# One attention phase on one core: a second load queue, a short first inverse, zeroing on GpSimd, and a new order of SyncE's work

## What is computed

```python
for t in range(S):
    y[:, :, t] = np.einsum('bhd,bhde->bhe', rt, state)
    Sa = np.einsum('bhde,bhe->bhd', state, at)
    state_decay = state * wt[:, :, None, :] - np.einsum('bhd,bhe->bhde', Sa, bt)
    state = state_decay + np.einsum('bhd,bhe->bhde', vt, kt)
```

## Time and profile before

| | us |
|---|---|
| median of 3 runs | 957.0 (953.57 to 958.44) |
| the profiled execution, its own time | 948.12 |
| its span, first to last instruction | 946.4 |
| TensorE busy | 801.0 (85%) |
| VectorE, ScalarE, GpSimd busy | 516.9, 384.4, 270.3 |

### The profile page before, as it was taken

The page is one execution under the profiler, slowest core; times in us unless marked ns, Lnnn a source line. Parts: engine busy times, 40 slices in busy tenths (PEclk is TensorE's granted clock), DMA queues, the critical chain, the costliest instruction groups (busy, mean ns, idle before and its releaser), DMA issues.

```text
span 946.4 us, 29782 instructions
## 1 busy us (share of the span) xinstructions
PE 801.0 (85%) x13477; PEld 740.6 (78%) x13477; DVE 516.9 (55%) x703; ACT 384.4 (41%) x511; POOL 270.3 (29%) x412
## 2 busy tenths in 40 slices
PE   2887299898998987778509998999989998999987
PEld 2776288787888876667508998999988998999987
DVE  5898076675756631222356348554476446763484
ACT  1222044443434333434336127652466317571264
POOL 1039881955918728200002020030201220020200
PEclk9987599999989896998858999999989999999999
DMA  9776565857555245341440000100101001010001
GB/s 104 116 119 107 82 93 121 121 96 132 96 89 98 52 95 154 69 68 32 138 140 1 1 21 14 59 1 1 34 1 59 1 1 34 17 43 1 1 1 42
DMA packets 229097, 58.04 MB, mean 61 GB/s; under 512 B 219728, under 2 KB 224364, under 8 KB 228972
## 3 DMA queue, kind: packets, MB, share of 16 engines
q1 hardware_dynamic: 202860, 52.21, 27.9%
q10 hardware_dynamic: 26112, 3.94, 2.8%
HBM read 41.96 MB, written 14.16 MB: 59 GB/s over the span
## 4 chain that ended last, share of the span: by engine, by line
PE 39%; DVE 5%; ACT 3%; DMA 2%; issue 1%; SPq 0%; DVEq 0%; ACTq 0%
PE pp L802 37%; DVE stage L1070 3%; PE pp L882 2%; ACT stage L975 1%; DVE w L990 1%; DVE big L990 1%; ACT stage L970 1%; DMA tmp<-in_moe_w_in_dram 1%; DMA rows_raw<-in_moe_conv_w_dram 1%; DMA tmp<-x_scratch 1%; ACT w L920 0%; ACT tmp L967 0%; SPq L729 0%; DMA out_dram<-stage 0%; ACT stage L985 0%
## 5 line engine op out<-in xcount | busy, mean ns | idle before, releaser
L246 POOL TENSOR_TENSOR prod<-t_pair 128x30 f32<-128x30 f32 (+9 forms) x180 | 105.0, 583 | 149.7 <-DMA t_pair<-m_scratch 135.9
L802 PE MATMUL pp<-xs,w 128*128 128x384 f32 x640 | 117.2, 339 | 0.2
L802 PEld LDWEIGHTS pp<-xs,w 128*128 128x128 f32 x640 | 112.8, 189 | 1.8 <-ACT stage L967 1.5
L249 POOL TENSOR_TENSOR t_pair<-t_pair,prod 128x30 f32<-128x30 f32 (+9 forms) x180 | 109.2, 607 | 14.1
L802 PE MATMUL pp<-wo,big 128*128 128x320 f32 x576 | 96.0, 327 | 13.0 <-DVE big L990 12.4
L802 PEld LDWEIGHTS pp<-wo,big 128*128 128x128 f32 x576 | 91.9, 201 | 16.0 <-issue 13.6
L802 PE MATMUL pp<-wsg,big 128*128 128x384 f32 x576 | 102.0, 338 | 0.0
L802 PEld LDWEIGHTS pp<-wsg,big 128*128 128x128 f32 x576 | 101.4, 188 | 0.0
L1088 POOL TENSOR_TENSOR big<-stage,big 128x1024 fp32r<-128x1024 f32 x12 | 28.8, 2397 | 253.7 <-DVE stage L1034 253.7
L348 DVE TENSOR_TENSOR ar_sb<-p,mask 128x512 f32<-128x512 f32 x24 | 16.6, 691 | 107.1 <-PE p L492 107.1
L802 PE MATMUL pp<-w,xs 128*128 128x512 f32 x192 | 47.6, 409 | 27.2 <-DVE xs L990 27.2
(11 more groups left out here) (128 smaller groups left out, 1479.3 us busy)
## 6 DMA issues: line engine op xcount, KB each, us to landing
vp<-in_v_dram ACTq DMA_DIRECT2D x96, 40.0 KB, 3.0
raw_r<-in_r_dram SPq DMA_DIRECT2D x48, 80.0 KB
x_scratch<-y_t SPq DMA_DIRECT2D x48, 80.0 KB
out_dram<-stage SPq DMA_DIRECT2D x12, 320.0 KB, 2.3
m_scratch<-n_t SPq DMA_DIRECT2D x48, 64.0 KB
t_pair<-m_scratch SPq DMA_DIRECT2D x6, 512.0 KB, 4.0
t_scratch<-t_pair SPq DMA_DIRECT2D x6, 512.0 KB, 4.4
t_sb<-t_scratch SPq DMA_DIRECT2D x24, 128.0 KB, 3.5
```

Source lines behind the costliest of these rows:

```text
L246: pool.tensor_tensor(p_v, tp[:, 0:s, s:s + 1].to_broadcast([PAIRS, s, n]), tp[:, s:s + 1, s + 1:C].to_broadcast([PAIRS, s, n]), ALU.mult). ...
L249: pool.tensor_tensor(tp[:, 0:s, s + 1:C], tp[:, 0:s, s + 1:C], p_v, ALU.add).then_inc(elim, 1)
L802: last = pe.matmul(out_of(p, half), l, r, start=step == 0 and first, stop=step == steps - 1 and not part)
```

## The change

It has four parts. (1) SyncE and ScalarE both load in the lead-in: k and a of the first two pairs of units and k of pairs 2 to 4 go out on ScalarE's queue, SyncE no longer waits for `padded`, and v's first loads go out in steps 5 and 6. (2) The sets are cut otherwise: set 0 holds units 0 and 1 only, the following ones four units each (2 to 5, 6 to 9, ...), the last one two, seven sets in place of six. Set 0 has 64 matrices, and each is split over two partitions, even rows on one and odd rows on the other. (3) GpSimd zeroes z, vp and r_t, and ScalarE the edge of w_back. (4) SyncE's list is put in another order: its iteration s now serves unit s - 1, beginning with the wait for that unit's n_t. LAG stays at 9. The diff, cut to its core:

```diff
+        SETS = NU // 4 + 1
+        T_OUT = [0] + [32 + 16 * g for g in range(SETS)]
+        M_IN = [0] + [64 + 16 * g for g in range(SETS)]
+        HEAD = 5
+        def set_of(u):
+            return (u + 2) // 4, (u + 2) % 4
+        def last_unit(g):
+            return min(4 * g + 1, NU - 1)
+        def first_chunk(g):
+            return max(4 * g - 2, 0)
+        t_first = free(s_sb[:], 0, [[C, C // 2], [1, C]])
         @block.sync
-            sp.wait_ge(padded, 9)
             load(w, "w", 0, w_in)
-            load(k, "k", 0, k_in)
             load(b, "b", 0, b_in)
-            load(a, "a", 0, a_in)
             load(w, "w", 1, w_in)
-            load(k, "k", 1, k_in)
             load(b, "b", 1, b_in)
-            load(a, "a", 1, a_in)
             load_r(0)
-            for s in STEPS:
+            for s in range(NC + LAG + 2):
+                u = unit(s - 1)
+                if u is not None:
+                    g, at = set_of(u)
+                    sp.wait_ge(n_done, 2 * u + 2)
...
+                    for be in range(2):
+                        n0 = be * HP + at * 16 if g else be * C + u * 16
+                        sp.dma_start(m_pairs[n0:n0 + 16].rearrange("n s t -> s n t"),
+                                     n_t[be * HP + C:be * HP + 2 * C, u % RN].rearrange("p j x t -> p (j x) t")).then_inc(m_out, 16)
+                    if u == last_unit(g):
+                        sp.wait_ge(m_out, (u + 1) * 32)
...
+                        if g == 0:
+                            for half in range(2):
+                                rows = slice(half * HP, (half + 1) * HP)
+                                sp.dma_start(t_first[rows], m_pairs[0:HP].rearrange("n (i x) t -> x n i t", x=2)[half]).then_inc(m_in, 16)
+                                sp.dma_start(t_pair[rows, 0], m_pairs[0:HP]).then_inc(m_in, 16)
+                        else:
+                            sp.dma_start(t_pair[:, g % 2], m_pairs).then_inc(m_in, 16)
+                for g in range(SETS):
+                    if s != first_chunk(g) + LAG - (1 if g else 2):
+                        continue
+                    sp.wait_ge(elim, ELIM[g + 1])
...
+                        sp.dma_start(t_pairs, t_pair[:, g % 2]).then_inc(t_out, 16)
+                    sp.wait_ge(t_out, T_OUT[g + 1])
...
+                cy = chunk(s - LAG - 2)
+                if cy is not None and cy % 2 == 1:
+                    sp.wait_ge(y_done, cy + 1)
...
+                        sp.dma_start(rows, y_t[bi * HP:bi * HP + D, :, be, :]).then_inc(y_out, 16)
                 if u is not None:
                     if u % 2 == 0 and u // 2 + 2 < NU // 2:
                         sp.wait_ge(w_full, u + 2)
                         load(w, "w", u // 2 + 2, w_in)
                     if u % 2 == 1 and u // 2 + 2 < NU // 2:
-                        sp.wait_ge(k_full, u + 1)
-                        load(k, "k", u // 2 + 2, k_in)
+                        if u // 2 + 2 >= HEAD:
+                            sp.wait_ge(k_full, u + 1)
+                            load(k, "k", u // 2 + 2, k_in)
                         sp.wait_ge(b_full, u + 1)
                         load(b, "b", u // 2 + 2, b_in)
                         sp.wait_ge(a_full, u + 1)
                         load(a, "a", u // 2 + 2, a_in)
-                ur = unit(s - R_LAG)
+                ur = unit(s - 1 - R_LAG)
                 if ur is not None and ur + 1 < NU:
                     sp.wait_ge(r_full, ur + 1)
                     load_r(ur + 1)
...
         @block.gpsimd
+            pool.wait_ge(mask_step, 5)
+            pool.memset(z[:], 0.0).then_inc(blank, 1)
+            pool.memset(vp[:], 0.0).then_inc(blank, 1)
+            pool.memset(r_t[:], 0.0).then_inc(blank, 1)
+            pool.wait_ge(m_in, M_IN[1])
+            for s in range(1, C - 1):
+                n, m = C - 1 - s, (s + 1) // 2
...
+                pool.tensor_tensor(p_v, t_first[:, 0:m, s:s + 1].to_broadcast([P, m, n]),
+                                   t_pair[:, 0, s:s + 1, s + 1:C].to_broadcast([P, m, n]), ALU.mult).then_inc(elim, 1)
...
         @block.scalar
+            load_side(k, "k", 0, k_in)
+            load_side(a, "a", 0, a_in)
             act.wait_ge(mask_step, 5)
-            for c in range(RV):
-                load_v(c)
+            act.activation(w_back[:, :, C - 1:C], mask[:, 0:16].rearrange("p (n o) -> p n o", o=1), ACT.Copy, scale=0.0)
...
+                if s == -1:
+                    load_side(k, "k", 1, k_in)
+                if s == 0:
+                    load_side(a, "a", 1, a_in)
+                if 5 <= s < 5 + RV:
+                    act.wait_ge(blank, 3)
+                    load_v(s - 5)
+                if 0 < s and s % 2 == 1 and s // 2 + 2 < HEAD:
+                    act.wait_ge(k_full, s + 1)
+                    load_side(k, "k", s // 2 + 2, k_in)
         @block.vector
-            dve.memset(w_back[:, :, C - 1:C], 0.0).then_inc(const_done, 1)
-            dve.memset(vp[:], 0.0)
-            dve.memset(r_t[:], 0.0)
-            dve.memset(z[:], 0.0).then_inc(const_done, 1)
         @block.tensor
-            pe.wait_ge(const_done, 4)
+            pe.wait_ge(padded, 9)
```

More of the change, by code:

```diff
@@ L147, in _ @@
             load(w, "w", 0, w_in)
-            load(k, "k", 0, k_in)
             load(b, "b", 0, b_in)
-            load(a, "a", 0, a_in)
             load(w, "w", 1, w_in)
-            load(k, "k", 1, k_in)
             load(b, "b", 1, b_in)
-            load(a, "a", 1, a_in)
             load_r(0)
-            for s in STEPS:
[L157 to L162, removed]
+            for s in range(NC + LAG + 2):
[3 more added lines that the diff above has]
+                    sp.wait_ge(n_done, 2 * u + 2)
+                    if g and at == 0:
+                        sp.wait_ge(m_in, M_IN[g])
+                    for be in range(2):
[4 more added lines that the diff above has]
+                        sp.wait_ge(m_out, (u + 1) * 32)
+                        if g >= 2:
+                            sp.wait_ge(t_out, T_OUT[g - 1])
+                        if g == 0:
[5 more added lines that the diff above has]
+                            sp.dma_start(t_pair[:, g % 2], m_pairs).then_inc(m_in, 16)
+                for g in range(SETS):
+                    if s != first_chunk(g) + LAG - (1 if g else 2):
+                        continue
+                    sp.wait_ge(elim, ELIM[g + 1])
+                    if g == 0:
+                        for half in range(2):
+                            sp.dma_start(t_pairs[0:HP].rearrange("n (i x) t -> x n i t", x=2)[half],
+                                         t_first[half * HP:(half + 1) * HP]).then_inc(t_out, 16)
+                    else:
@@ L173, in _ @@
+                cy = chunk(s - LAG - 2)
+                if cy is not None and cy % 2 == 1:
+                    sp.wait_ge(y_done, cy + 1)
+                    for be, bi in SIDES:
+                        rows = x_t[2 * bi + be].rearrange("(h e) s -> e h s", e=D)[:, :, (cy - 1) * C:(cy + 1) * C]
+                        sp.dma_start(rows, y_t[bi * HP:bi * HP + D, :, be, :]).then_inc(y_out, 16)
                 if u is not None:
@@ L191, in _ @@
                     load_r(ur + 1)
[L192 to L213, removed]
+                if s == NU + 1:
+                    sp.wait_ge(scanned, 2 * NU)
+                    sp.dma_start(staged, to_stage).then_inc(stage_in, 16)
             sp.wait_ge(y_out, 16 * 4 * (NC // 2))
@@ L235, in _ @@
                                    pattern=[[1, C]], channel_multiplier=-1).then_inc(mask_step, 1)
-            for g in range(NU // 4):
+            pool.wait_ge(mask_step, 5)
[3 more added lines that the diff above has]
+            pool.wait_ge(m_in, M_IN[1])
+            done = 0
+            for s in range(1, C - 1):
+                n, m = C - 1 - s, (s + 1) // 2
+                p_v = prod[:, 0:m * n].rearrange("p (j t) -> p j t", t=n)
+                if done:
+                    pool.wait_ge(elim, done)
+                pool.tensor_tensor(p_v, t_first[:, 0:m, s:s + 1].to_broadcast([P, m, n]),
+                                   t_pair[:, 0, s:s + 1, s + 1:C].to_broadcast([P, m, n]), ALU.mult).then_inc(elim, 1)
+                pool.wait_ge(elim, done + 1)
+                pool.tensor_tensor(t_first[:, 0:m, s + 1:C], t_first[:, 0:m, s + 1:C], p_v, ALU.add).then_inc(elim, 1)
+                done += 2
+            for half in range(2):
+                pool.wait_ge(elim, done + half)
+                pool.memset(free(s_sb[half * HP:(half + 1) * HP], half, [[C + 2, C // 2]]), 1.0).then_inc(elim, 1)
+            for g in range(1, SETS):
                 tp = t_pair[:, g % 2]
-                pool.wait_ge(m_in, (g + 1) * 16)
-                done = g * ELIM
+                pool.wait_ge(m_in, M_IN[g + 1])
+                done = ELIM[g]
                 for s in range(1, C - 1):
```

43 lines of the change are left out of this document (27 added, 16 removed).

## The result

The changed kernel took 986.8 us (median of 3, 986.06 to 987.45) against 957.0: a ratio of 1.032 with a 95% interval of [1.027, 1.036]. The profiled execution has a span of 985.7 against 946.4, 39.3 more, at a mean granted clock of 0.900 of full speed against 0.925.

The account below looks back on a forecast made before the run. TensorE was taken as the bound, any hold-up paid in full. 948.1 less 0.95 and 6.5 gained, plus 43.8 of late r loads, gives 984.5 us; times 1.0094, a median of 994, range of 8 in 10 from 955 to 1015.

Parts of the forecast that it names:

- Lead-in: Start of the kernel: first scan at 10.1 us, first G at 16.7, 6.65 earlier than before.
- Set 0: First inverse on GpSimd: starts at 38.3, takes 29.7 us, ends at 68.0; removes the 21 us wait at chunk 0.
- The mean gap per operation: Set 0 on GpSimd: 21.4 us by elements, 29.7 with the mean gap of the two earlier sets shown.
- Step 9: Last step before step 10: r late by some 4 us behind k, b and a, swallowed by step 10's wait.
- Step 10: r queues behind set 1's end: its transposes at 128.8, before 135.3; 6.5 of the 28 us gained are left.
- The six late loads: Even steps 12 to 22: r, last in SyncE's order, late by 4.0, 13.8 or 4.2 us, 43.8 in all.
- Sum: Whole kernel, profiled execution: 948.1 - 0.95 - 6.5 + 43.8 = 984.5 us; times 1.0094, a median of 994.
- Rival 1: Even steps: r comes in time, T of set 1 decides, 22 us gained: 925, median 934; chance 0.15.
- Rival 2: TensorE's gaps and slack swallow part of each wait, step 10 at its lower bound: 962 to 973; chance 0.07.
- rival 3: SyncE: T's store queues behind the set's load, each round trip some 3 us longer: above 1015; chance 0.03.
- The threshold "SyncE sends r off within 10 us of n_t": SyncE's iterations: the prediction is wrong if r's load goes out within 10 us of n_t.
- the element rate of the prediction: GpSimd's set operations: 0.163 us each plus 0.00224 per element.

Follow-up runs that it names:

- one_queue: r_first with all lead-in loads back on SyncE's queue, in the old order w, k, b, a: 935.14 us, 0.987 of the kernel before.
- r_first: The changed kernel with r's load moved to the head of each SyncE iteration, ahead of the wait for n_t: 938.95 us, 0.989 of the kernel before.
- r_y_first: r_first with y's stores also moved ahead of T's round trip: 928.34 us, 0.980 of the kernel before.
- order_alone: The kernel before with only SyncE's list put in the new order; old sets, lead-in loads and zeroing kept: 1002.1 us, 1.055 of the kernel before.
- y_between: The changed kernel with y's stores moved ahead of T's round trip, r's load still last: 983.43 us, 1.038 of the kernel before.
- the four fastest orders: r_y_first (0.980); that with w ahead of T (0.978); this with two loads of a on ScalarE's queue (0.977); the changed kernel in SyncE's old order (0.983).
- unsplit: r_y_first with set 0 eliminated as whole matrices on 64 partitions, one load and one store of the set: 937.27 us, 0.982 of the kernel before.

## Why the prediction was right

The direction, the mechanism and the range held: 987 lies in 955 to 1015, 7 us below the 994 forecast. By its own steps:

- **Lead-in.** First scan 10.72 (forecast 10.1), first G 17.22 (16.7). The two-queue load is worth nothing that these runs can tell: one_queue shows it directly. The rule of the Trainium skill (Trainium Kernel Development and Optimization, Key Constraints), that issuing from several engines saves only issue time, said as much, and the runs agree (0.987 with one queue, 0.989 with two). That the scan comes 2 us earlier on one queue and G does not was not foreseen.
- **Set 0 is the mis-sized term of the gain.** It started at 36.69, 1.6 before the forecast, and took 36.2 us, not 29.7; it ended at 72.9, not 68.0. Set 1 took 39.0 (40.3) and ended at 111.9 (108.3). The mean gap per operation, taken from two sets that met 7 and 3 of VectorE's scans, did not hold for one that met 10; the last section shows it. For chunk 0 it was in time all the same.
- **Step 9** was held up as well by w (7.71 us), a wait that the prediction left out; w's load stood behind T of set 0, which came 4.9 us late. r was late by 4.5 (4). As forecast, nothing of it reaches the end, because step 10 waits for set 1.
- **Step 10**: 111.9 + 7.8 (T's round trip) + 8.4 (k, b, a) + 1.7 + 2.4 is 132.2, 132.3 without rounding, forecast 128.8: all of the difference is set 1's end. The wait was 13.8 us instead of 17, since step 9 had been late.
- **The six late loads**: 4.56, 4.54 and 5.12 in steps 12, 16 and 20 (4.0 each); 13.66 and 12.05 in 14 and 18 (13.8); 5.25 in 22 (4.2); 45.2 in all, forecast 43.8. This near a hit is partly luck. In step 14 r was issued and landed 29.7 us behind n_t (27.4 forecast): the stretch from m's stores to y's took 17.9 us (14.0), T's store having landed later; the 12 loads took 8.1 (9.6). And TensorE came to r 16.1 us after n_t's end (185.05 to 201.1) and not after 13.6. Two terms 2.3 to 2.5 too small cancel.
- **Sum.** 984.5 in terms of the profiled execution, which measured 987.45: 3 too low. Step 10 makes 3.5 of it and the late loads 1.4, and some 2 came back, since the time grew by less than the waits' sum. The forecast of the median is 7 us too high all the same because of the factor 1.0094 by which I went from there to the median: it added 9. It took for granted that the changed kernel's profiled execution, too, would lie 0.9% below its median; it lay at it. The profiled executions stand 39.3 us apart and the medians 29.8; the 957.0 of before lies above its medians on the other chips (947.5 to 956.0). So the 7 us are a sum 3 too low and a factor 9 too high, which partly cancel; the range held either way.
- **Rivals.** Rival 1 (r in time) is what r_first makes true by another way. Its price was 925 in terms of the profiled execution; r_first's took 937.65, since y's stores and set 1's T came in r's place, and r_y_first's 929.18. Rival 2 (the waits swallowed) is out: in order_alone r's waits came to 63.8 us, T's fell by 8.2, and the time rose by 52, so that some 4 us were swallowed; in the changed kernel it was 2. Of rival 3 a piece is there: the store's landing took 5.7 us in the median where it was 3.7 with y's stores between. Yet y_between shows that this decides nothing: the order in which r stands last absorbs it.
- The threshold "SyncE sends r off within 10 us of n_t" was the right test: it was 12.5 in step 12 (n_t ended at 149.8, r was issued at 162.2) and 26 in step 14.

What stays open: whether splitting set 0 pays at the end of the kernel, which of the dropped waits makes the lead-in's gain, and which of the four fastest orders is best; these runs tell none of it.

## What to carry to other kernels

An engine's DMA list is worked through in order: put first what is due first, and behind it whatever waits for another engine or for a store's landing; sum the issue times and waits ahead of each load and compare them with the time between its release and its use. When a change frees a wait of 20 us, ask what each queue has to do by the new, earlier time: here one part saved 22 us for chunk 0 and another, in the same change, asked for 45 us in pieces of 4 to 14. Undo the parts one by one before you reject a change; three of its four parts were worth 1.8% together.

## What the hardware showed that I had not expected

**A VectorE scan costs the GpSimd operation that meets it about 0.8 us, whether the operation is short or long.** The order in time of the changed kernel, the first operations of set 0, and VectorE in the same stretch:

```profile
37.94 0.28 POOL L280 TENSOR_TENSOR prod<-s_sb,t_pair 128x56 f32<-128x56 f32 x1
38.30 1.11 POOL L283 TENSOR_TENSOR s_sb<-s_sb,prod 128x56 f32<-128x56 f32 x1
39.49 1.08 POOL L280 TENSOR_TENSOR prod<-s_sb,t_pair 128x54 f32<-128x54 f32 x1
40.65 0.29 POOL L283 TENSOR_TENSOR s_sb<-s_sb,prod 128x54 f32<-128x54 f32 x1
```

```profile
38.11 1.22 DVE L418 TENSOR_TENSOR_SCAN e_scan<-w_fore,stage 128x512 f32<-128x512 f32 x1
39.24 1.26 DVE L442 TENSOR_TENSOR_SCAN r_scan<-w_back,stage 128x512 f32<-128x512 f32 x1
```

The two GpSimd operations that meet the scans take 1.11 and 1.08 us where their neighbours of the same size take 0.28 and 0.29, and end within 0.1 us of the scans (39.33, 40.50). In set 0 ten of the 60 are stretched like this (1.08 to 1.46), and five more, each under an e_t product, to 0.70 to 0.84. The first set of before has longer operations, up to 0.70. There, where they meet a scan:

```profile
82.53 0.69 POOL L249 TENSOR_TENSOR t_pair<-t_pair,prod 128x240 f32<-128x240 f32 x1
83.30 1.47 POOL L246 TENSOR_TENSOR prod<-t_pair 128x240 f32<-128x240 f32 x1
84.85 1.45 POOL L249 TENSOR_TENSOR t_pair<-t_pair,prod 128x240 f32<-128x240 f32 x1
```

```profile
83.15 1.21 DVE L352 TENSOR_TENSOR_SCAN e_scan<-w_fore,stage 128x512 f32<-128x512 f32 x1
84.28 1.57 DVE L376 TENSOR_TENSOR_SCAN r_scan<-w_back,stage 128x512 f32<-128x512 f32 x1
```

1.47 and 1.45 against 0.69: the loss is about 0.8 again, and the second scan takes longer too (1.57 against 1.21). So what counts is how many scans a set meets. Windows over set 0 of the changed kernel and over the first set of before (columns as in the earlier trace rows):

```profile
36.69:72.92 36.23, 26.66 (x290) 23.26 (x289) 35.44 (x54) 8.82 (x15) 31.49 (x62) 0.99 1.08 128
```

```profile
61.95:103.60 41.65, 24.73 (x332) 22.27 (x330) 28.31 (x40) 8.57 (x15) 37.01 (x61) 0.76 0.49 83
```

And over the unsplit set 0 (unsplit):

```profile
33.94:80.23 46.29, 35.16 (x388) 31.77 (x388) 43.53 (x60) 10.70 (x18) 41.66 (x61) 0.85 0.77 100
```

By the element rate of the prediction set 0 should have kept GpSimd busy for 21.4 us and did for 31.5, 10.1 more; the first set of before 32.0 and did for 37.0, 5.0 more. The first met 10 scans and 5 e_t products, with VectorE busy 98% of the stretch; the second 7 and 4 at 68%, since in its last 12 us, while TensorE waited for T, only one scan began. The unsplit set 0 is the fair comparison: VectorE was busy 94% of its 46.3 us, it met 12 scans and 6 e_t products, and GpSimd was busy for 41.7 against 32.0 by elements, 9.7 more. Split or not, the collisions cost about 10 us, and the split kept nearly the whole gain of 10.6 by elements (36.2 against 46.3 us). The prediction's error of 6.5 us was to carry over a mean gap per operation from sets that met fewer scans. The Trainium skill (SBUF — State Buffer, "Who interferes with whom") gives a rule for it: a VectorE instruction with two SBUF inputs contends with a GpSimd instruction that reads SBUF, while one with at most one SBUF input does not, outside its two-port modes. The trace agrees in what it shows: the scans and e_t (both inputs in SBUF) stretch GpSimd's operations, while a_t's and kb_t's, with p as an input, pass beside unstretched ones.

**A second queue can delay the first tile.** w's transposes start at 8.33 with k beside it on ScalarE's queue and at 6.33 when w goes out alone on SyncE's (one_queue), and G is no earlier for it.

**TensorE ran below full speed behind waits of 4.5 us, and its gaps paid for part of it.** Windows of the changed kernel behind the waits of step 9 and of step 12 (columns as in the earlier trace rows):

```profile
102.20:112.00 9.80, 9.68 (x258) 8.58 (x258) 2.08 (x3) 3.56 (x7) 8.33 (x20) 0.64 0.20 57
166.53:183.42 16.89, 16.73 (x460) 14.99 (x460) 7.37 (x10) 6.40 (x10) 0.00 (x0) 0.78 0.23 40
```

A granted clock of 0.64 and 0.78 is a mixture of 2.4 and 1.2 GHz; what preceded them were idle times of 4.53 and 4.56 us. The transposes of r behind such a wait take 1.11 and not the 0.66 of a calm step. A stretch without a wait was at 1.00. The prediction had put this at nothing, because TensorE's gaps of 1.7 us a step might give as much back. They did in part: in the second window TensorE is busy 16.7 us of 16.9, where the same step before has 13.9 of 15.6, so that the step is 1.3 us longer and not 2.9. From r's transposes in step 10 to those in step 23 the changed kernel took 246.8 us, the kernel before 203.8: 43.0 more, for 45.2 us of waits. The seven steps behind the waits were 3.2 us longer than before, and the six with a wait, less the wait, 5.4 us shorter; why these are shorter no run separates.
